# Moving key conversions, one transpose, one subtraction and one wait in a fused attention, MLP and mixture-of-experts kernel

## What is computed

```python
scores = scale * np.matmul(q, k.transpose(0, 1, 3, 2))
kth = np.partition(scores, -32, axis=-1)[..., -32:-31]
scores = np.where(scores >= kth, scores, -1e9)
attn = softmax(scores)                      # over the 32 kept keys
x = np.matmul(attn, v)                      # reshaped to 1152 x 512
h = x @ w_in                                # 512 -> 2048
x2 = (np.maximum(h, 0) + alpha * np.minimum(h, 0)) @ w_out
top2 = two best of 8 experts by noisy gate logits of x2
out[token] = sum over its two experts of weight * (relu(x2 @ w1[e]) @ w2[e])
```

## Time and profile before

| | |
|---|---|
| median of 3 runs | 721.94 us (720.70 to 722.93) |
| profiled execution, its own time | 721.94 us |
| its span, first to last instruction | 720.2 us |
| PE busy | 660.1 us, 92% of the span |
| DVE, ACT, POOL busy | 529.9, 466.9, 393.0 us |
| mean granted TensorE clock | 0.979 of full speed |

### The profile page before, as it was taken

The page is one execution under the profiler, slowest core; times in us unless marked ns, Lnnn a source line. Parts: engine busy times, 40 slices in busy tenths (PEclk is TensorE's granted clock), DMA queues, the critical chain, the costliest instruction groups (busy, mean ns, idle before and its releaser), DMA issues.

```text
span 720.2 us, 13740 instructions
## 1 busy us (share of the span) xinstructions
PE 660.1 (92%) x4690; PEld 560.7 (78%) x4690; DVE 529.9 (74%) x1111; ACT 466.9 (65%) x880; POOL 393.0 (55%) x436
## 2 busy tenths in 40 slices
PE   2467789999999999999999999899999999999994
PEld 2356668877877788888888778688998989989893
DVE  5999999999688989898998453785455555555521
ACT  5788878787888787787777745845454553545511
POOL 3598899887888777678767757221130311303022
PEclk9987989999999999999999999999999999999998
DMA  9879438546418435364462787745845728457222
GB/s 294 355 257 394 133 149 293 207 162 216 162 33 280 179 133 202 106 249 163 174 236 94 301 334 250 257 149 177 283 112 197 234 91 288 112 194 218 91 37 36
DMA packets 39964, 141.01 MB, mean 196 GB/s; under 512 B 11152, under 2 KB 12176, under 8 KB 35856
## 3 DMA queue, kind: packets, MB, share of 16 engines
q1 hardware_dynamic: 35520, 130.25, 50.7%
q0 software_dynamic: 4384, 9.98, 6.2%
HBM read 113.70 MB, written 45.73 MB: 221 GB/s over the span
## 4 chain that ended last, share of the span: by engine, by line
PE 70%; POOL 10%; ACT 7%; DVE 5%; issue 4%; DMA 2%; POOLq 0%; another core or an unknown queue 0%; SPq 0%; ACTq 0%; DVEq 0%
PE bank L1280 11%; PE bank L1090 10%; PE ps_scores L1264 9%; PE bank L1053 7%; PE bank L1029 6%; PE bank L1264 6%; PE bank L1285 4%; PE bank L1058 3%; PE ps_scores L980 3%; PE bank L1011 3%; POOL w_in_parts L1797 2%; POOL expo L1785 2%; DMA k_raw<-kt_in_dram 2%; POOL k_parts L1742 2%; PE bank L1070 2%
## 5 line engine op out<-in xcount | busy, mean ns | idle before, releaser
L440 DVE MAX8 top<-rest 128x8 f32<-128x576 f32 x216 | 152.2, 745 | 0.0
L1937 POOL DMA_INDIRECT out_dram<-ye,xe x24 | 42.8, 1785 | 190.0 <-ACT ye L1683 164.5
L1785 POOL TENSOR_TENSOR expo<-scores,expo 128x576 f32<-128x576 f32 x72 | 103.7, 1441 | 49.1 <-ACT scores L1373 49.0
L452 DVE MATCH_REPLACE8 rest<-top,rest 128x576 f32<-128x576 f32 x144 | 105.7, 741 | 0.0
L1090 PE MATMUL bank<-w_out_high,g_parts 128*128 128x512 f32 x288 | 99.9, 407 | 0.8 <-issue 0.6
L663 DVE TENSOR_TENSOR w_lo<-raw,w_hi 128x1024 fp32r<-128x1024 f32 x64 | 78.2, 1225 | 20.3 <-ACT w_hi L1610 19.3
L1280 PE MATMUL bank<-w_hi,he_t 128*128 128x512 f32 x224 | 80.8, 401 | 1.4 <-DVE he_t L732 1.4
L1029 PEld LDWEIGHTS bank<-v,prob_t 128*64 128x64 f32 (+1 forms) x1440 | 56.9, 144 | 29.9 <-ACT prob_t L1400 15.3
L1029 PE MATMUL bank<-v,prob_t 128*64 128x65 f32 (+1 forms) x1440 | 72.5, 240 | 5.5 <-ACT prob_t L1400 5.4
L1610 ACT CAST w_hi<-raw 128x1024 fp32r<-128x1024 f32 x64 | 66.9, 1046 | 7.5 <-DMA raw<-w_dram 7.4
L1264 PE MATMUL ps_scores<-xe_t,w_hi 128*128 128x320 f32 x320 | 70.8, 308 | 0.0
(11 more groups left out here) (244 smaller groups left out, 1621.1 us busy)
## 6 DMA issues: line engine op xcount, KB each, us to landing
raw<-w_dram SPq DMA_DIRECT2D x64, 512.0 KB, 11.9
w_in_parts<-w_parts_dram SPq DMA_DIRECT2D x14, 2048.0 KB, 7.9
x_sorted_dram<-x_sorted_dram SPq DMA_DIRECT2D x7, 2570.0 KB, 10.7
w_parts_dram<-w_in_parts SPq DMA_DIRECT2D x4, 2048.0 KB, 10.0
q_raw<-q_rows_dram SPq DMA_DIRECT2D x18, 256.0 KB, 4.7
w_in_raw<-w_in_dram SPq DMA_DIRECT2D x4, 1024.0 KB, 11.2
w_out_raw<-w_out_dram SPq DMA_DIRECT2D x4, 1024.0 KB, 13.8
w_lo<-w_parts_dram SPq DMA_DIRECT2D x2, 2048.0 KB, 13.4
```

The lines of the kernel that those rows point to most:

```text
L440: nc.vector.max(dst, src).then_inc(chain if r < ROUNDS - 1 else dve_top, 1)
L452: nc.vector.match_replace(rest[:, k, :], top[:, (n + k) % 4, 8 * r:8 * r + 8], src, LOWEST).then_inc(chain, 1)
L1785: nc.gpsimd.tensor_tensor(expo[:, n % 4, :], scores[:, n % SBUFS, :], expo[:, n % 4, :], ALU.mult).then_inc(pool_prob, 1)
```

## The change

Five edits, none of which adds or removes arithmetic.

1. ACT: high parts of keys 0, 1, 2, 4 and 6 now stand ahead of the tile's copy of the scores (new table K_HIGH_AT), those of 3, 5 and 7 behind the exponentials, where all stood before; the tiles are 22, 24, 29, 29, 30, 30, 31, 31 for keys 0 to 7, instead of 23, 25, 27, 28, 29, 30, 31, 33.
2. POOL: low parts at tiles 24, 26, 30, 30, 31, 31, 32, 32, instead of 24, 26, 28, 29, 30, 31, 32, 34; those of keys 3, 5 and 7 behind the prelu or low_g of the tile, after a wait for that step.
3. PE: in the mixed block at head 2 the h_transpose stands behind the scores, as elsewhere.
4. POOL: low_g stands ahead of normalise. The two meet at head 1 of each block from block 2 on.
5. POOL: the wait for y_added and the count of ye_free now follow the last item too.

```diff
-K_HIGH_BEHIND = {23: 0, 25: 1, 27: 2, 28: 3, 29: 4, 30: 5, 31: 6, 33: 7}
-K_LOW_AT = {24: 0, 26: 1, 28: 2, 29: 3, 30: 4, 31: 5, 32: 6, 34: 7}
+K_HIGH_AT = {22: 0, 24: 1, 29: 2, 30: 4, 31: 6}
+K_HIGH_BEHIND = {29: 3, 30: 5, 31: 7}
+K_LOW_AT = {24: 0, 26: 1, 30: 2, 31: 4, 32: 6}
+K_LOW_BEHIND = {30: 3, 31: 5, 32: 7}
...
-                    late_scores = mixed_block and h == 2
-                    if late_scores:
-                        h_transpose(blk - 1, TURN_AT[h])
...
-                    if mlp and h in TURN_AT and not late_scores:
+                    if mlp and h in TURN_AT:
                         h_transpose(blk - 1, TURN_AT[h])
...
+                    if isinstance(tile, int) and tile in K_HIGH_AT:
+                        second_high_keys(K_HIGH_AT[tile])
                     if not first and not (last and h + AHEAD >= HEADS):
                         copy_scores(tile + AHEAD, h + AHEAD)
...
-                    if mlp and h == (1 if after_mixed else 0):
-
-                        normalise(blk - 1, 0)
-                    if mlp and h == 1 and blk > 1:
-                        normalise(blk - 1, 1)
                     if rest and h in REST_LOW_AT:
                         low_g(blk - 2, REST_LOW_AT[h])
                     if mlp and h in LOW_AT:
                         low_g(blk - 1, LOW_AT[h])
+                    if mlp and h == (1 if after_mixed else 0):
+
+                        normalise(blk - 1, 0)
+                    if mlp and h == 1 and blk > 1:
+                        normalise(blk - 1, 1)
...
+                    if isinstance(blk, int) and HEADS * blk + h in K_LOW_BEHIND:
+                        if h in LOW_AT:
+                            pool.wait_ge(pool_g_low, 4 * (blk - 1) + LOW_AT[h] + 1)
+                        elif h in PRELU_AT:
+                            pool.wait_ge(pool_g, 4 * (blk - 1) + PRELU_AT[h] + 1)
+                        else:
+                            pool.wait_ge(pool_g, 4 * (blk - 2) + REST_PRELU_AT[h] + 1)
+                        low_keys(1, K_LOW_BEHIND[HEADS * blk + h])
...
-                if not last:
-                    pool.wait_ge(y_added, 48 * g + 48)
-                    pool.sem_inc(ye_free, 1)
+                pool.wait_ge(y_added, 48 * g + 48)
+                pool.sem_inc(ye_free, 1)
```

More of the change, by code:

```diff
@@ L1837, in one_block @@
                         low_keys(1, K_LOW_AT[HEADS * blk + h])
+                    if rest and h in REST_LOW_AT:
+                        low_g(blk - 2, REST_LOW_AT[h])
+                    if mlp and h in LOW_AT:
+                        low_g(blk - 1, LOW_AT[h])
                     if mlp and h == (1 if after_mixed else 0):
@@ L1842, in one_block @@
                         normalise(blk - 1, 1)
[L1843 to L1846, removed]
                     if rest and h in REST_PRELU_AT:
```

## The result

The changed kernel took 726.37 us, median of 4 runs (724.51 to 726.61), against 721.88 of the kernel before (720.70 to 722.93): a ratio of 1.0061, 95% interval 1.0043 to 1.0080, that is 4.5 us more (3.1 to 5.8). It is slower by about 0.6%.

The account below looks back on a forecast made before the run. PE bounds the kernel, busy throughout except 3.5 us idle from 150 to 218 us. Terms 1.27 (low_g, block 2) + 0 (blocks 5 to 8) + 0.75 (keys) + 0.85 (exit) = 2.87 on 721.94 give 724.8 us, range 721.6 to 727.6.

Parts of the forecast that it names:

- low_g in block 2, +1.27: Tile 17: low_g ahead of normalise holds back PE's x_transpose, and the delay goes through: 1.27 us more.
- Blocks 5 to 8, 0: Steady blocks: normalise has 1.68 us before x_transpose's weight load, so low_g ahead of it costs 0, some 0.35 left.
- The keys with low_g in blocks 3 and 4, +0.75: Tiles 22 to 34: PE gains 1.33 up to tile 32, then pays it back; +0.75 us, bounds -1.5 and +2.
- Together +0.75: Sum of the walk through the keys' tiles 22 to 34, booked as the price of moving the keys: +0.75 us.
- ACT's crowd at tiles 29 to 32: ACT's stretch between these tiles' prob_t holds six keys, not three: 21.2 us instead of 17.06, with 1.8 of buffer waits.
- The exit, +0.85: Kernel end: POOL's DRAIN starts only after the last landing and takes 2.5 us, so the end comes 0.85 us later.
- The bounds of 0.2 and 5.6: Length of POOL's DRAIN at the exit: from 0.18 (end 1.45 us sooner) to 5.6 us (end 3.95 later).
- ACT and POOL keep up: Rival, tiles 31 to 33: PE keeps its 1.33 us gain, exit unchanged, 721.7 us; chance 0.15.
- A short DRAIN: Rival at the exit: the end comes 1.45 us sooner, total +0.57, 722.5 us; chance 0.12.
- one of 5.6 us: Rival at the exit: POOL's DRAIN costs its full 3.95 us, total +5.97, 727.9 us; chance 0.15.
- the keys and the exit do nothing: Rival: PE feels nothing of the key moves or exit wait, only block 2's 1.27, 723.2 us; chance 0.13.

Follow-up runs that it names:

- e_lowg: The kernel before with only low_g ahead of normalise on POOL, in every block: 724.26 against 721.81 us, ratio 1.0040.
- after_again: The changed kernel, unchanged, timed and traced once more against the kernel before: 726.63 against 722.21 us, ratio 1.0059.
- x_b2: The kernel before with low_g ahead of normalise in block 2 alone: 722.49 against 721.09 us, ratio 1.0016.
- x_b5: The kernel before with low_g ahead of normalise only in blocks 5 and later: 721.54 against 721.09 us, ratio 1.0007.
- e_keys: The kernel before with only the new key tables and the mixed block's h_transpose behind the scores: 721.59 against 721.81 us, ratio 1.0000.
- e_nowait: The changed kernel with the old exit, without POOL's wait after the last item: 723.58 against the kernel before's 721.81 us, ratio 1.0026.

## Why the prediction was right, and where it was not

The forecast was 724.8 us with a range of 721.6 to 727.6, slower the likeliest; it is 726.4. Where the sum had 2.87 us, 3.75 can be seen (2.0 of PE's delay and 1.75 of the exit); the rest up to the measured 4.5, some 0.7 us, is inside the interval of the measurement (3.1 to 5.8) and not placed.

- **low_g in block 2, +1.27: right.** 1.26 and 1.30 in the traces of e_lowg and after_again, 1.2 us by the times of x_b2. (In three other traces the clock hides it, see the last section.)
- **Blocks 5 to 8, 0: right.** In x_b5 the weight load comes 0.40 behind normalise; less the 0.06 of the hand-over that is 0.34, where I had read 0.35.
- **The keys with low_g in blocks 3 and 4, +0.75: right in size, walked correctly but for two tiles, and put down to the wrong edit.** Counted from behind block 2, after_again has +0.8 at block 3's x_transpose (predicted 0.87), +0.5 at tile 27 (0.49), -1.35 at tile 30 (-0.93), -1.2 at tile 32 (-1.33), +0.9 at the h_transpose of tile 32 (0.73), +1.05 at tile 33 (0.9), +0.7 from 257 us on (0.75). The two misses on the way nearly cancel: tile 30 wins 0.4 more than I had walked, but the wait at tile 32, of which I had 0.4 go, is 0.68. At tile 34 0.35 goes, where I had 0.15. But the step that failed is "Together +0.75" as the price of the keys: of what stands behind block 2, the swap of low_g alone makes 1.6 (e_lowg, 2.89 - 1.27), the tables with the h_transpose 0.00, and with the swap in place they take 0.9 off. I had asked of the swap what it costs in block 2 and in blocks 5 to 8, and left out that blocks 3 and 4 have the same POOL order and as little slack: in block 3 PE even waits 0.21 for normalise, and in block 4 normalise ends at 210.83 and x_transpose starts at 210.89, just as in the earlier trace rows. A row that I had used for the keys held the price of the other edit.
- **ACT's crowd at tiles 29 to 32: right.** Four waits of 2.14 (predicted 1.8), 207.65 - 186.14 = 21.51 from prob_t of tile 29 to prob_t of tile 32 (21.2).
- **The exit, +0.85: right in kind, mis-sized.** 3.51 us of DRAIN where I took 2.5, so +1.75. The bounds of 0.2 and 5.6 held. I took the 1.75 behind the landing for the DRAIN's own work and added a little; the 3.5 was hidden in the trace of before, beside the transfer. The rule of the Trainium skill that I had set beside it (VectorE: DVE Perf Modes, The DRAIN you can't avoid: some 12 ns on all engines) is of no use for POOL's exit here: 3507 ns in three traces with nothing in flight. The section speaks of the DRAINs that the runtime adds, and these carry a line of the kernel, L122, so it may not be meant for them. Nor was the 0.18 us of POOL's DRAIN at the start a measure for the one at the end.
- **The rivals.** That ACT and POOL keep up is out (tile 32). A short DRAIN and one of 5.6 us are out. That the keys and the exit do nothing is out for the exit; for the keys alone a balance of 0 is what e_keys shows, by gains and losses that cancel and not by waits that sit elsewhere.

## What to carry to other kernels

Where an edit has the same form in several blocks, price every block, by the slack between the held-back instruction and its reader: 0.06 of slack is 1.27 lost, 1.68 is nothing, and edits that share an engine are to be priced together, since here 2.9 and 0 made 2.0. A conversion that goes through one buffer is to be spread one to a tile, behind what the bottleneck will ask for next: the same eight keys came out at 0 crowded, with 0.35 of help from the h_transpose, and earned 2.6 us spread. And a wait that only repeats what another engine already waits for can still cost: it keeps POOL from beginning its exit under the transfer.

## What the hardware showed that I had not expected

**POOL's exit has 3.5 us of its own in this kernel, where its last work is indirect DMAs, and they hide under a transfer.** 3507 ns when it starts at the landing, an end 1.75 us behind the landing when it starts 2 us or more ahead. POOL's last DMA instruction ends long before that: 714.37 against a landing at 718.2. The Trainium skill (Perfetto Trace Analysis, DMA Instruction — SWDGE (GPSIMD)) says the same of such rows: the end that the profiler shows is that of the descriptors, not of the data. The traces agree, 3.8 us apart.

**The granted clock differs from run to run, and it changes where an edit is paid.** Stretches of x_b2 and then of e_lowg, columns as in the earlier trace rows, the granted clock third from the end:

```profile
98.00:102.00 4.00, 4.00 (x41) 3.40 (x40) 4.00 (x5) 2.73 (x7) 3.92 (x3) 1.00 0.18 66
102.00:106.00 4.00, 1.28 (x7) 0.72 (x5) 4.00 (x11) 2.52 (x4) 4.00 (x4) 1.00 0.15 66
106.00:108.00 2.00, 2.00 (x10) 1.96 (x11) 2.00 (x5) 0.84 (x3) 1.68 (x5) 0.56 1.17 492
```

```profile
98.00:102.00 4.00, 4.00 (x32) 3.42 (x30) 4.00 (x5) 2.92 (x8) 3.92 (x4) 0.50 0.18 66
102.00:106.00 4.00, 3.80 (x17) 2.80 (x15) 4.00 (x11) 2.35 (x4) 3.96 (x4) 0.84 0.31 131
106.00:108.00 2.00, 2.00 (x14) 1.82 (x14) 2.00 (x5) 1.37 (x4) 1.72 (x4) 1.00 0.94 393
```

The program is the same up to here, and DVE, which is busy throughout, sets the pace. In x_b2 the granted clock is 1.00 (2.4 GHz) at 98 to 102, PE is done early, idles 2.72 us, and then gets about half (1.2 GHz) until about 110: it comes out 1.6 us later than in the trace of before (PE's delay, here not counted from tile 17, goes from 0.27 at 105.7 to 1.86 at 110.6). In e_lowg, as in the trace of before, it has 0.50 first, hardly idles, and has the full clock when work comes. The changed kernel's first trace, e_nowait and x_b2 are of the first sort. In them the x_transpose of block 2 comes no more than 0.4 later, counted from tile 17 (-0.2, 0.2 and 0.4), as PE is already late; the 1.27 is not on top of the clock's 1.6, but mostly under it. One trace of such a kernel can thus make a cost vanish or appear, which is why the delays above are counted in several.
